# First two tiles loaded as plain rows and turned on TensorE, spatial weights turned on VectorE, a looser order in mixing and tail

## The reference

```python
B, H, S, D = 2, 8, 768, 64           # attention; n_global 8, n_local 96
scores = q @ k.T / sqrt(D) + bias; a = softmax(where(keep, scores, -1e9)); x = a @ v   # x: (2, 768, 512)
h = relu(x @ w_in); u, v = h[..., :512], h[..., 512:]          # w_in 512 x 1024
v_s = einsum('ts,bsd->btd', w_spatial, layernorm(v)) + b_spatial[None, :, None]
x = (u * v_s) @ w_out
u = x + (x.T @ U @ V).T                                        # rank 32
out = u + relu(u @ w_ch1) @ w_ch2                              # 512 -> 2048 -> 512
```

## Time and profile before

| | us |
|---|---|
| median of three runs (lowest, highest) | 562.88 (561.10, 563.14) |
| the profiled execution | 561.43 |
| its span, first to last instruction | 559.6 |
| TensorE busy in the span | 525.5 (94%) |
| VectorE busy | 292.0 (52%) |
| ScalarE busy | 172.2 (31%) |
| GpSimd busy | 112.1 (20%) |

### The profile page before, as it was taken

How to read it: one execution, slowest core, us unless ns; L and a number is a source line. 1 busy time by engine, 2 the same in 40 slices (tenths; PEclk the granted TensorE clock), 3 DMA queues, 4 the chain that set the end, 5 groups by cost and what they waited for, 6 DMA issues and landing times.

```text
span 559.6 us, 7557 instructions
## 1 busy us (share of the span) xinstructions
PE 525.5 (94%) x2676; PEld 409.6 (73%) x2676; DVE 292.0 (52%) x848; ACT 172.2 (31%) x426; POOL 112.1 (20%) x134
## 2 busy tenths in 40 slices
PE   1778999989999999999989999999999999999996
PEld 0455666567777788878768888888888888888885
DVE  4778888867775535689822265523146524011112
ACT  2665665555555533232311101021110102111010
POOL 3886000000000001499389500000000000000000
PEclk9999999999999999999989999999999999999999
DMA  8996453555514100055223100002000002000002
GB/s 176 220 222 131 101 103 90 119 113 131 127 48 123 29 29 1 1 170 166 79 75 114 37 1 0 1 0 76 0 1 1 1 0 77 0 1 0 1 0 81
DMA packets 43979, 37.04 MB, mean 66 GB/s; under 512 B 25600, under 2 KB 37888, under 8 KB 43936
## 3 DMA queue, kind: packets, MB, share of 16 engines
q1 hardware_dynamic: 37920, 20.13, 16.8%
q0 software_dynamic: 3216, 11.63, 6.8%
q10 hardware_dynamic: 2800, 4.72, 2.9%
HBM read 33.33 MB, written 3.15 MB: 65 GB/s over the span
## 4 chain that ended last, share of the span: by engine, by line
PE 80%; DVE 9%; DMA 3%; POOL 3%; issue 3%; ACT 1%; SPq 0%; DVEq 0%; POOLq 0%; ACTq 0%
PE ps L1185 66%; PE ps L1177 5%; PE ps L1225 4%; PE ps L1200 4%; DMA w_raw<-in_moe_w_in 3%; DVE uT_first L1003 2%; POOL win_lo L433 2%; PE ps L1316 1%; DMA qk_even<-in_q 1%; POOL win_hi L431 1%; DVE pr L875 1%; DVE uT_lo L1010 1%; DVE wspT_lo L962 1%; DVE gv_lo L943 1%; DVE sc L859 1%
## 5 line engine op out<-in xcount | busy, mean ns | idle before, releaser
L1123 DVE SCALAR_TENSOR_TENSOR hT_lo<-ps,hT_hi 128x512 fp32r<-128x512 f32 x48 | 33.2, 692 | 171.4 <-ACT hT_hi L731 171.4
L731 ACT ACTIVATE hT_hi<-ps 128x512 fp32r<-128x512 f32 x48 | 28.7, 598 | 228.3 <-PE ps L1185 228.3
L557 ACT ACTIVATE pr<-sc,small 128x256 f32<-128x256 f32 (+1 forms) x96 | 46.2, 483 | 52.5 <-DVE small L859 52.0
L1200 PE MATMUL ps<-k_turned,q_turned 64*128 64x256 f32 (+1 forms) x192 | 35.4, 448 | 16.5 <-DVE k_turned L811 10.0
L859 DVE CUSTOM_DVE_ANT_0 sc<-ps,bias 128x256 f32<-128x256 f32 (+1 forms) x96 | 34.9, 399 | 19.7 <-PE ps L1200 16.3
L1185 PE MATMUL ps<-win_hi,xT_hi 128*128 128x512 f32 x96 | 39.9, 416 | 0.0
L1003 DVE STREAM_TRANSPOSE ys<-tokens 32x128 f32<-32x128 f32 x128 | 38.7, 302 | 1.8
L1185 PE MATMUL ps<-uT_hi,w1a_hi 128*128 128x512 f32 x96 | 38.0, 396 | 1.0 <-DVE uT_lo L1010 1.0
L1185 PE MATMUL ps<-uT_hi,w1a_lo 128*128 128x512 f32 x96 | 38.1, 396 | 0.0
L1185 PE MATMUL ps<-uT_lo,w1a_hi 128*128 128x512 f32 x96 | 38.0, 396 | 0.0
L1185 PE MATMUL ps<-win_hi,xT_lo 128*128 128x512 f32 x96 | 37.7, 393 | 0.0
(11 more groups left out here) (146 smaller groups left out, 1078.0 us busy)
## 6 DMA issues: line engine op xcount, KB each, us to landing
w_raw<-in_moe_w_ch POOLq DMA_DIRECT2D x16, 512.0 KB, 4.0
wsp<-in_moe_w_spatial ACTq DMA_DIRECT2D x12, 384.0 KB, 3.5
vn<-in_v SPq DMA_DIRECT2D x12, 256.0 KB, 3.8
out<-ys SPq DMA_DIRECT2D x12, 256.0 KB, 3.3
qk_late<-in_q SPq DMA_DIRECT2D x24, 112.0 KB, 3.5
qk_late<-in_k SPq DMA_DIRECT2D x24, 112.0 KB, 3.9
vp<-in_v SPq DMA_DIRECT2D x10, 224.0 KB, 4.5
w_raw<-in_moe_w_in POOLq DMA_DIRECT2D x4, 512.0 KB, 7.1
```

Source lines behind the costliest of these rows:

```text
L557: act.activation(pr[:, k % 3, e, 0:w], sc[:, k % 2, e, 0:w], ACT.Exp, bias=nmax[:, k % 2, e:e + 1], scale=-1.0, accum_out=sums[:, k % 3, e ...
L731: act.activation(hT[0][:, n % 2, :], h1_ps(n), ACT.Relu).then_inc(s["hT_hi"], 1)
L1123: dve.scalar_tensor_tensor(hT[1][:, n % 2, :], h1_ps(n), 0.0, hT[0][:, n % 2, :], ALU.max, ALU.subtract).then_inc(s["hT_lo"], 1)
L1200: pe.matmul(scores_ps(e)[:, 0:w], q_turned[rows, tile % 2, p, :], keys[:, window_at(i):window_at(i) + w]).then_inc(s["scores"], 1)
```

## The change

- **First tiles.** q and k of tiles 0 and 1 come as plain rows, one transfer of 256 KB for each (`load_first`, 256-byte pieces as v has them). TensorE turns them with four transposes each (`turn_first`). ScalarE copies q0, k0 and q1 out of PSUM (`set_first`), VectorE copies k1 (`set_first_keys`). VectorE's `turn` begins with tile 2.
- **Scores.** The first eight units have two PSUM homes (`FOUR`). Products of the identity with itself, whose results nobody reads, are added ahead of and in the first units (`keep_busy`).
- **Chunks of w_in.** GpSimd asks for chunk 0 without waiting for q, and for chunk 1 when chunk 0 has landed.
- **Spatial weights.** They are loaded by four transfers to a tile in 128-byte pieces, so that VectorE turns half a tile by one `dve.transpose` of 128x384 (`turn_wsp`). It writes to the room of `wspT_lo`; ScalarE and VectorE split it from there. In batch 1 odd tiles have a home of their own. The 72 transposes on TensorE go.
- **PSUM homes.** Turned probabilities have two homes up to unit 30, x up to tile 7 (`PAIRED`).
- **Order in the mixing of batch 0.** `project` stands behind the third unit, `gate_transpose` behind the second. On VectorE `gT_lo` stands behind the third unit.
- **Batch 1.** The last three parts of the input product stand as v(4), v(5), u(4), u(5) (`u_v_late`). Eight of the sixteen groups of `turn_tokens` go ahead into the layer norms; in `products(1)` the spatial weights are turned and split ahead of `gate`, and `uT_lo` comes one tile sooner.
- **Tail.** `hidden(0)` stands ahead of `low_rank(1, 4)`.

```diff
+FOUR = 8
+WARM = 5
+PAIRED = (ALONE + NP) // NP
...
+        wsp_turned = sb("wsp_turned", [P, NT, P])
...
+        def scores_ps(k, e):
+            return ps[:, (2 * (k % 2) if k < FOUR else 0) + e, :]
...
+        wsp_d = w_sp.rearrange("(i r a) (k y c) -> i y r (a k) c", a=TURNS, r=TURN, y=TURNS, c=TURN)
...
+        def load_first(e, tile, a):
+            e.dma_start(qk_first[tile][:, a, :, :],
+                        (q_first_d, k_first_d)[a][0, tile, :, :, :]).then_inc(s["qk"[a] + qk_signal(tile)], 16)
...
-            pool.wait_ge(s["q_loaded0"], 64)
             load_chunk(0)
+            pool.wait_ge(s["chunk_loaded0"], 16)
             load_chunk(1)
...
+            def set_first(tile, a, dst):
+                act.wait_ge(s["first_turned"], 2 * tile + a + 1)
+                act.activation(dst, turned_first(tile, a), ACT.Copy).then_inc(s["first_set"], 1)
...
-            turn(0, q_turned[:, 0, :, :])
+            def set_first_keys():
+                dve.wait_ge(s["first_turned"], 4)
+                dve.tensor_copy(k_turned[:, :, 1, 0:P], turned_first(1, 1))
+                dve.wait_ge(s["first_set"], 2)
+                dve.tensor_copy(k_turned[:, :, 0, P:SLOT], k_turned[:, :, 0, 0:G]).then_inc(s["qk_turned"], 1)
...
+            def turn_wsp(b, t, h):
+                m = b * NT + t
+                half = slice(h * HALF, (h + 1) * HALF)
+                if h == 0:
+                    loads = sum(wsp_second(n // NT, n % NT) == wsp_second(b, t) for n in range(m + 1))
+                    dve.wait_ge(s[f"wsp_loaded{int(wsp_second(b, t))}"], 16 * TURNS * loads)
+                    dve.wait_ge(s["mixed"], m - 1 if b and t else m)
+                dve.transpose(wsp_turned_of(b, t)[:, half, :].rearrange("p k (r a) -> p a k r", a=TURNS),
+                              wsp_in(b, t)[:, :, half, :]).then_inc(s["wsp_turned"], 1)
...
-                dve.tensor_tensor(lo, wsp_ps(h, wide), hi, ALU.subtract).then_inc(s["wspT_lo"], 1)
+                dve.tensor_tensor(wspT_of(b, t)[1][:, half, :], wsp_turned_of(b, t)[:, half, :], wspT_of(b, t)[0][:, half, :],
+                                  ALU.subtract).then_inc(s["wspT_lo"], 1)
...
@@ VectorE, products(b)
+                    if t + 1 < NT:
+                        for h in range(2):
+                            turn_wsp(b, t + 1, h)
+                        for h in range(2):
+                            wsp_lo(b, t + 1, h)
+                    if b:
+                        gate(b, t, True)
+                        if t < TB:
+                            for g in (8 + 2 * t, 9 + 2 * t):
+                                turn_tokens(g // TURNS, g % TURNS)
...
@@ VectorE, window(), mixing of batch 0
+                    unit(a, True)
                     if t:
                         x2_lo(0, t - 1, False)
-                    unit(a, True)
                     turn_next(a)
                     gate(0, t, False)
+                    turn_wsp(after, (t + 1) % NT, 0)
                     unit(a + 1, True)
-                    gT_lo(0, t)
+                    turn_wsp(after, (t + 1) % NT, 1)
                     turn_next(a + 1)
-                    wsp_lo(after, (t + 1) % NT, 0, False)
+                    wsp_lo(after, (t + 1) % NT, 0)
                     if a + 2 <= LAST:
                         unit(a + 2, True)
+                        gT_lo(0, t)
                         turn_next(a + 2)
...
@@ VectorE, window(), layer norms of batch 1
                     layer_norm(1, t)
+                    if t <= TB:
+                        for g in (2 * t - 2, 2 * t - 1):
+                            turn_tokens(g // TURNS, g % TURNS)
...
@@ TensorE
+            def keep_busy(k, n):
+                for _ in range(n):
+                    pe.matmul(idle_ps(k), ident[:, :], ident[:, :])
...
-                wait(pe, "biased", 2 * k)
+                wait(pe, "biased", 2 * (k - 1 if 0 < k < FOUR else k))
...
+            def u_v_late(b, t, wide):
+                for q in (0, 1):
+                    u_v_piece(b, t, q, wide)
+                for q in (2, 3):
+                    if t == NT - 1:
+                        u_v_piece(b, t - 1, q, wide)
+                for q in (2, 3):
+                    if t != NT - 2:
+                        u_v_piece(b, t, q, wide)
...
@@ finish()
                 products(1)
-                wait(pe, "wspT_lo", 2 * B * NT)
+                hidden(0)
                 low_rank(1, NT - 2, True)
-                hidden(0)
```

More of the change, by code:

```diff
@@ L754, in _ @@
         def _(dve):
-            give(dve, "qk_turned", "bias_ready", "biased", "normal", "xT_lo", "d_xT_lo", "wspT_lo", "gate", "gT_lo",
+            give(dve, "qk_turned", "bias_ready", "biased", "normal", "xT_lo", "d_xT_lo", "gate", "gT_lo",
                  "x2_split", "mix_split", "u_ready", "hT_lo", "y_ready")
+            dve.sem_inc(s["qk_turned"], 1)
             steps = [0]
@@ L1024, in products @@
                     gT_lo(b, t)
-                    for x in range(2, TURNS):
-                        if b and t < TB:
-                            turn_tokens(t, x)
-                    if b and t >= 2:
-                        uT_lo(0, t - 2)
+                    if b and 0 < t <= TB:
+                        uT_lo(0, t - 1)
             def every():
@@ L1219, in probs_v @@
                     pe.wait_ge(s[f"v_loaded{buf}"], 16 * values_loaded(tile))
-                    wait(pe, "xT_lo", tile if tile > NT else tile - 1)
+                    wait(pe, "xT_lo", tile if tile > PAIRED else tile - 1)
                 values = [vp, vn] if tile % NT else [vn]
```

252 lines of the change are left out of this document (160 added, 92 removed).

## The result

| | before | after |
|---|---|---|
| median (lowest, highest), us | 562.70 (561.10, 563.14) | 569.28 (567.41, 571.13) |
| ratio, 95% interval | 1 | 1.0122 [1.0077, 1.0167] |
| profiled execution, its span | 561.43, 559.6 | 571.13, 569.2 |
| VectorE busy in the span | 292.0 | 311.5 |
| mean granted clock | 0.995 | 0.970 |

Slower by 6.6 us, where 4.9 us faster was forecast. To see where, I cut each profiled execution at five starts on TensorE: the first product of the mixing of batch 0, u_v(1, 0), the first and the last `gate_transpose` of batch 1, and `hidden(0)`. From `hidden(0)` to the end of the span it was 272.6 us before and 270.9 after.

What follows compares the result with a forecast made beforehand. TensorE was taken to bound the kernel from 37 us on, with VectorE close beside it. The terms summed to -4.9 on the profiled 561.43, 556.5; with 1.45 for the median, 558.0 us, range 543 to 566.

Steps and rivals of the forecast that it cites:

- start, to the first product: Kernel start: chunk 0 asked for sooner and units earlier bring the first w_in product forward; -5.3 us, between 0 and -6.5.
- end of the attention: Attention's end with the input product: second home of x removes a wait, VectorE gains transposes; -1.9 us, from -3.3 to 0.
- mixing of batch 0: Transposes leave TensorE, but it waits for VectorE's longer queue, mostly in tile 0; +4.0 us, between -4.4 and +7.
- layer norms, first mixing tile of batch 1: VectorE's added transposes and splits overrun its free time and delay the first gate_transpose; +5.3 us, between -1.2 and +7.5.
- mixing of batch 1: Later mixing tiles: TensorE loses its transposes and VectorE's queue fits within its time; -3.0 us, from -3.5 to +2.
- tail: End of batch 1's mixing: hidden(0) directly follows the last gate_transpose, without slow stretch; -4.0 us, between -2 and -4.5.
- rival C: Batch 1: GpSimd's splits hold VectorE's wspT_lo, which now reads SBUF twice; slower, 566.2 us; chance 0.15.
- The slow clock: TensorE throttled behind the longer wait ahead of 246 us, in batch 1; 1.2 us, left out of the sum.

Runs made afterwards that it cites:

- turns back: Changed kernel with the eight groups of turn_tokens moved from the layer norms of batch 1 back into its mixing; 571.93 us, ratio 1.0141.
- the kernel of 554.8 us: Changed kernel with the order of the mixing of batch 0 taken back and GpSimd's last-stage weight splits begun behind batch 1's fourth gate; 554.79 us, ratio 0.9878.
- Late splits: Changed kernel with GpSimd's splits of the last stage's weights begun behind the fourth gate of batch 1; 561.09 us in a single execution.

## Why the prediction was wrong

Against the terms of the sum, from the table. For the first two I took the medians over the profiles: with the old start (three) the first product stands at 37.7 and the mixing of batch 0 at 119.0, with the new one (twelve, three of them with small edits there) at 34.5 and 114.3.

| step | predicted | measured |
|---|---|---|
| start, to the first product | -5.3 | -3.2 |
| end of the attention | -1.9 | -1.5 |
| mixing of batch 0 | +4.0 | +6.2 |
| layer norms, first mixing tile of batch 1 | +5.3 | +7.3 |
| mixing of batch 1 | -3.0 | +1.1 |
| tail | -4.0 | -3.5, and 1.7 less behind `hidden(0)` |

- **Start.** The mechanism was right, the size was not: chunk 0 landed after 6.2 us and not 4.7, and GpSimd needed 23.9 us and not 22.15. In two of the twelve profiles the gain was lost again by the end of the attention, in the changed kernel's own (118.6) and in that of turns back (118.0). In both GpSimd's `TENSOR_TENSOR` meets `pr` at 47 us, TensorE waits 2.0 us, and its clock falls behind that. The meeting alone does not do it: the kernel of 554.8 us had it too (1.78 us for one `pr`, a wait of 1.69), its clock stayed at 1.00, and its mixing began at 113.5.
- **Mixing of batch 0.** The waits came where they were laid out. Tile 0 took 4.9 us more than before where 2.9 were forecast; its waits sum to 3.95 us, as forecast (4.0), and most of the difference is the term left out, the lower clock behind them. Tile 4 took 1.7 more and not 0.8, with a wait of 1.46 for `gT_lo`; the other four lie within 0.4 of the forecast. In the five profiles with this order the stage took 87.4 to 91.0 us, so +6.2 is the least of them; with their median, 88.5, the terms measured add up to +5.8, where the medians of the runs differ by 6.6.
- **Layer norms and mixing of batch 1.** This is the step that failed. The forecast took `wspT_lo` at 0.5 us, its duration out of PSUM, and kept the held ones for rival C at 0.15; five of ten took 1.3 to 2.7 us. Late splits give 4.0 us back in the first stage and 1.7 in the second, against 1.4 and 0.1 in the kernel before, so 4.2 of the 6.1 us by which the two terms missed are C. What is left lies in the second stage. There the five tiles from gate to gate took 43.5 us; five free ones of 7.74 would be 38.7, near the 39.4 of the forecast. Above that stand 1.6 us in the first tile, at the lower clock, and 1.7 and 1.5 in the second and third, with the waits of 1.58 and 1.30 for `gated` behind held splits. With late splits these two go, but the first tile at the lower clock takes 2.4 over 7.74 and not 1.6, so the 1.7 of the table is less than what C cost here.
- **C's own price** was right: +7.5 at the first term (7.3 measured), -3.0 + 4.8 at the second (+1.1), 1.2 for the slow clock. It made 566.2, and with the start and the end of the attention as measured 568.7; that this is within 1 us of 569.3 is in part luck, as it has the mixing of batch 0 at 4.0.
- **Tail.** Right, to 0.2 us when done alone (3.8 us, with an interval of about 1.4 to each side).
- **The slow clock** was named in the prediction and left out of the sum, although showed it behind two waits of 1.56 and 1.00 us. A wait of 4 us that one predicts is a reason to put it in.

The direction was wrong for these reasons together: with C gone alone a single execution took 561.1 us, no clear gain yet, and only with the order of batch 0 taken back as well did the time reach 554.8. The two PSUM homes and the order of the late input product were not varied by themselves; their share of the -1.5 and of the layer norms stays open.

C deserved more than 0.15: the changed kernel read SBUF twice in the stretch in which the earlier trace rows had shown 2.09 us for such an instruction.

## What to carry over

When an edit moves an operand from PSUM to SBUF, or work onto VectorE, look first which engine works in the same stretch; price the instruction by the held row of its kind, not by the free one. Work for a later stage that an idle engine does early (here GpSimd's splits) is not free: start it as late as its reader allows. And a predicted wait on TensorE is priced with what its clock may take afterwards, 1.4 to 3.4 us where it fell in a tile or behind `hidden(0)`; in a queue, what the next stage waits for stands ahead of anything that itself waits.
